# A linear-attention recurrence run seven slots ahead instead of six, with its input loads split and its VectorE and ScalarE order changed

## The reference

```python
for t in range(S):                       # S = 768, D = 40, 4 x 8 heads
    y[:, :, t] = np.einsum('bhd,bhde->bhe', rt, state)
    Sa = np.einsum('bhde,bhe->bhd', state, at)
    state_decay = state * wt[:, :, None, :] - np.einsum('bhd,bhe->bhde', Sa, bt)
    state = state_decay + np.einsum('bhd,bhe->bhde', vt, kt)
```

## Time and profile before

| | |
|---|---|
| median of 3 runs | 1002.68 us (999.1 to 1007.23) |
| the profiled execution | 1005.59 us, its span 1003.9 us |
| busy over the span | PE 82%, DVE 55%, ACT 31%, POOL 25% |
| recurrence | from 0 to about 441 us of the span |
| mean granted TensorE clock | 0.83 of full speed from 104 to 383 us, 0.99 after 435 us |

### The profile page before, as it was taken

One profiled execution on the slowest core, in us unless ns is written; L12 is line 12 of the kernel. 1 busy time (PEld: TensorE's weight loads), 2 busy tenths in 40 slices (PEclk: granted clock), 3 DMA queues, 4 the chain that ended last, 5 costly groups with the idle time before them and its releaser, 6 DMA issues.

```text
span 1003.9 us, 27604 instructions
## 1 busy us (share of the span) xinstructions
PE 826.9 (82%) x11872; PEld 603.9 (60%) x11872; DVE 556.5 (55%) x1235; ACT 312.4 (31%) x739; POOL 252.2 (25%) x524
## 2 busy tenths in 40 slices
PE   2318988897998978859998789997899987899977
PEld 2218888897887978844454555455544545554555
DVE  8686667767776653125436635347355366353464
ACT  3102222223222222212225532235422255312354
POOL 1075856687776876000000000000000000000000
PEclk9999787898777888789999999999999999999999
DMA  3525455565656536232000000100000000000000
GB/s 102 137 57 115 96 131 127 131 147 112 137 121 132 133 73 159 60 101 81 10 31 7 21 14 1 40 1 21 14 7 30 10 12 17 14 1 0 1 21 20
DMA packets 125336, 61.31 MB, mean 61 GB/s; under 512 B 105120, under 2 KB 118048, under 8 KB 123296
## 3 DMA queue, kind: packets, MB, share of 16 engines
q1 hardware_dynamic: 95172, 32.61, 14.5%
q10 hardware_dynamic: 30044, 26.94, 10.4%
HBM read 45.37 MB, written 14.16 MB: 59 GB/s over the span
## 4 chain that ended last, share of the span: by engine, by line
PE 66%; DVE 15%; DMA 7%; ACT 6%; issue 4%; SPq 2%; ACTq 1%; DVEq 0%
PE ps_all L737 9%; PE ps_all L721 8%; PE ps_scan L103 4%; PE ps_all L778 4%; DMA l_by_unit<-l_blocks 3%; PE ps_all L854 3%; PE ps_all L815 3%; PE ps_scan L194 3%; ACT probs L914 3%; PE ps_scan L174 3%; PE ps_all L833 3%; PE ps_all L731 3%; PE ps_all L845 2%; PE ps_all L724 2%; DVE t_update_first L314 2%
## 5 line engine op out<-in xcount | busy, mean ns | idle before, releaser
L314 POOL TENSOR_TENSOR t_update<-l_by_unit,t_by_unit 128x133 f32<-128x133 f32 (+13 forms) x251 | 118.0, 470 | 131.8 <-DVE t_by_unit L316 64.4
L316 POOL TENSOR_TENSOR t_by_unit<-t_by_unit,t_update 128x133 f32<-128x133 f32 (+13 forms) x251 | 128.8, 513 | 19.7
L103 PE MATMUL ps_scan<-decayed_a_and_eye,scaled_then_x 40*128 40x104 f32 x768 | 67.8, 346 | 55.9 <-DVE decayed_a_and_eye L346 55.9
L721 PE MATMUL ps_all<-scaled_then_x,inputs_then_w_up 128*128 128x384 f32 x256 | 91.0, 499 | 15.7 <-DMA scaled_then_x<-y_t 10.0
L103 PEld LDWEIGHTS ps_scan<-decayed_a_and_eye,scaled_then_x 40*128 40x128 f32 x768 | 62.7, 252 | 57.9 <-DVE decayed_a_and_eye L346 42.3
L1005 DVE TENSOR_REDUCE minus_max<-ps_all 128x1 f32<-128x128 f32 (+5 forms) x96 | 54.9, 618 | 75.2 <-PE ps_all L819 75.2
L737 PE MATMUL ps_all<-gated,w_down 128*128 128x384 f32 x256 | 91.1, 499 | 0.0
L721 PEld LDWEIGHTS ps_all<-scaled_then_x,inputs_then_w_up 128*128 128x128 f32 x256 | 48.7, 194 | 52.2 <-issue 12.0
L880 ACT ACTIVATE h<-ps_all 128x384 f32<-128x384 f32 x64 | 28.0, 490 | 148.7 <-PE ps_all L724 148.7
L737 PEld LDWEIGHTS ps_all<-gated,w_down 128*128 128x128 f32 x256 | 46.0, 189 | 44.6 <-issue 19.1
L951 DVE TENSOR_SCALAR conv<-h,w_conv 128x768 f32<-128x768 f32 x32 | 19.9, 621 | 94.7 <-ACT h L880 94.7
(11 more groups left out here) (115 smaller groups left out, 1519.2 us busy)
## 6 DMA issues: line engine op xcount, KB each, us to landing
inputs_then_w_up<-in_x ACTq DMA_DIRECT2D x46, 321.4 KB
r_t_and_v_t<-in_rv ACTq DMA_DIRECT2D x48, 160.0 KB
l_by_unit<-l_blocks SPq DMA_DIRECT2D x24, 256.0 KB, 5.0
uv_and_ruv<-in_v ACTq DMA_DIRECT2D x48, 80.0 KB, 3.0
y_t<-y_out SPq DMA_DIRECT2D x24, 160.0 KB
out<-out_rows SPq DMA_DIRECT2D x24, 160.0 KB, 1.8
l_blocks<-ak_and_l SPq DMA_DIRECT2D x96, 32.0 KB, 2.0
t_blocks<-t_by_unit SPq DMA_DIRECT2D x24, 128.0 KB, 4.7
```

The lines of the kernel that those rows point to most:

```text
L103: last = nc.tensor.matmul(PS[:, o:o + ROWS], weights, AL[c % NK][rows(h), p, :], start=True, stop=True)
L314: return (lambda: eng.tensor_tensor(tmp[:, 0:cols, 0:rest], l[:, s:s + 1, s + 1:BLK].broadcast_to(shape), t[:, 0:cols, s:s + 1].broadcast_ ...
L316: lambda: eng.tensor_tensor(t[:, 0:cols, s + 1:BLK], t[:, 0:cols, s + 1:BLK], tmp[:, 0:cols, 0:rest], ALU.subtract))
L721: nc.tensor.matmul(bank[n][:, 0:HALF], WIN[:, t, cols], XT[:, t, n * HALF:(n + 1) * HALF], start=(t == 0), stop=False)
```

## The change

GA becomes 7, so a chunk is prepared seven slots ahead, the loop has one slot more ahead of slot 0, and one more buffer of three kinds is allocated (by NK and NQK). A chunk's input load becomes three parts with semaphores of their own: w, a, and k with b. On ACT the w part of the next chunk is issued after the copy of x, the a part of this slot's chunk after that of y, the k and b part of the next chunk after `bkn_move`, and the second copy of x (`ZS`) stands ahead of `bkn_move`. On DVE the odd slots have a new order: four solver steps, hm, five solver steps, gm, prefixes, suffixes, bk and the rest. Even slots keep theirs. `solve_first` moves to slot -3, at the same chunks as before.

```diff
-GA = 6
+GA = 7
+FIRST = 4
+PARTS = {"w": slice(0, WCOLS + 1), "a": slice(WCOLS + 1, WCOLS + 1 + HC), "kb": slice(WCOLS + 1 + HC, XCOLS)}
...
-        def load_x(c):
+        def load_x(c, part):
             if c >= 2:
                 act.wait_ge(m["prepped"], c - 1)
             for h in range(2):
-                act.dma_start(INX[c % 2][rows(h), :], in_x[c, h]).then_inc(m[f"inx{c % 2}"], 16)
+                act.dma_start(INX[c % 2][rows(h), PARTS[part]], in_x[c, h][:, PARTS[part]]).then_inc(m[f"{part}{c % 2}"], 16)
...
             if live: move(XS, PX, "x", "x_sb", n)
+            if next_up: load_x(n + GA + 1, "w")
             if live: move(YS, PY, "y", "y_sb", n, -1.0)
-            if 2 <= n + GA + 1 < NT: load_x(n + GA + 1)
+            if soon: load_x(n + GA, "a")
+            if live: move(ZS, PX, "e", "z_sb", n)
             if ahead: bkn_move(c)
-            if live: move(ZS, PX, "e", "z_sb", n)
+            if next_up: load_x(n + GA + 1, "kb")
             if live: u_move(n)
...
-            if prep: prefixes(c)
-            if after: hm(n - 1)
-            if prep: suffixes(c)
-            if n % 2 == 1 and 2 <= (n + GA - 3) // 2 < NPAIR: solve_head((n + GA - 3) // 2)
-            if ahead: gm(g)
-            if n == -2: solve_first()
+            pair = (n + 3) // 2
+            if n % 2 == 1 and 2 <= pair < NPAIR:
+                solve_head(pair, range(0, FIRST))
+                hm(n - 1)
+                solve_head(pair, range(FIRST, HEAD))
+                if ahead: gm(g)
+                if prep: prefixes(c)
+                if prep: suffixes(c)
+            else:
+                if prep: prefixes(c)
+                if after: hm(n - 1)
+                if prep: suffixes(c)
+                if ahead: gm(g)
+            if n == -3: solve_first()
```

More of the change, by code:

```diff
@@ L72, in recurrence @@
              "solved pool_chain set_eye consts set_inx set_dve set_pool arrived go "
-             "inx0 inx1 v0 v1 v2 r0 r1 r2 l_out0 l_out1 l_in t_out t_in0 t_in1 stored0 stored1")
+             "w0 w1 a0 a1 kb0 kb1 v0 v1 v2 r0 r1 r2 l_out0 l_out1 l_in t_out t_in0 t_in1 stored0 stored1")
     m = {n: sem("r_" + n) for n in names.split()}
@@ L266, in scalar @@
         act.wait_ge(m["set_inx"], 2)
-        load_x(1)
+        for part in ("w", "kb", "a"):
+            load_x(1, part)
         act.wait_ge(m["consts"], 4)
@@ L279, in scalar @@
             live, ahead = 0 <= n < NT, 0 <= c < NT
+            soon, next_up = 2 <= n + GA < NT, 2 <= n + GA + 1 < NT
             if live: move(XS, PX, "x", "x_sb", n)
+            if next_up: load_x(n + GA + 1, "w")
             if live: move(YS, PY, "y", "y_sb", n, -1.0)
-            if 2 <= n + GA + 1 < NT: load_x(n + GA + 1)
+            if soon: load_x(n + GA, "a")
+            if live: move(ZS, PX, "e", "z_sb", n)
             if ahead: bkn_move(c)
-            if live: move(ZS, PX, "e", "z_sb", n)
+            if next_up: load_x(n + GA + 1, "kb")
             if live: u_move(n)
@@ L321, in prefixes @@
         def prefixes(c):
-            dve.wait_ge(m[f"inx{c % 2}"], 32 * (c // 2 + 1))
+            dve.wait_ge(m[f"w{c % 2}"], 32 * (c // 2 + 1))
             if c >= 1:
@@ L334, in bk @@
         def bk(c):
+            dve.wait_ge(m[f"kb{c % 2}"], 32 * (c // 2 + 1))
             if c >= 2:
@@ L342, in al @@
         def al(c):
+            dve.wait_ge(m[f"a{c % 2}"], 32 * (c // 2 + 1))
             if c >= NK:
@@ L388, in solve_first, with solve_head @@
                     sub().then_inc(m["solved"], 1)
[L390 to L396, removed]
+        def solve_head(j, steps):
+            if steps.start == 0:
+                dve.wait_ge(m["l_in"], 32 * (j + 1))
+                dve.wait_ge(m["eye"], j + 1)
+                dve.wait_ge(m["solved"], 1)
+                if j >= 3:
+                    dve.wait_ge(m["head"], j - 2)
+            for s in steps:
                 mult, sub = step(nc.vector, LU[j % 2], TS[j % 2], TMD, s)
@@ L527, in sync @@
         sp.wait_ge(m["set_inx"], 1)
-        for h in range(2):
-            sp.dma_start(INX[0][rows(h), :], in_x[0, h]).then_inc(m["inx0"], 16)
+        for part in ("w", "kb", "a"):
+            for h in range(2):
+                sp.dma_start(INX[0][rows(h), PARTS[part]], in_x[0, h][:, PARTS[part]]).then_inc(m[f"{part}0"], 16)
         sp.wait_ge(m["set_pool"], 1)
```

## The result

The changed kernel is **slower, by 1.4%**: median 1020.6 us over 20 runs (1007.95 to 1030.41), the kernel before 1001.7 over 20 (994.47 to 1009.24), ratio 1.014 with a 95% interval of 1.010 to 1.017. Runs more than 1.5% above the fastest of the same kernel, 8 of the 20 here and none of the kernel before, are left out of this and all later ratios; the plain medians give 1.019. Forecast were 980 us and a range that ended at 1001.

The account below looks back on a forecast made before the run. PE work plus low clock was taken as the bound, with DVE's l_in wait lengthening odd slots. Pairs fall from 31.6 to 28.4 us, 29 less; start costs 7.2, slot 18 gives 1: 23 less, 980 us, range 955 to 1001.

Parts of the forecast that it names:

- the first of the odd slots: DVE, odd slots: four solver steps follow al's end at +3.6 directly, take 1.91 us and end at +5.5.
- the 6.0 us that the prediction took off each odd slot: Odd slots: gm starts at g_products' end, +10.6 and not +16.6, so 6.0 us less each at full clock.
- the queue behind the head's wait: Rival: DVE's head still waits for l_in, hm and g_products behind it; about 998 us, 1009 at worst; chance 0.08.
- l_in's waits: DVE's eight waits for l_in, 26.4 us, go; the round trip fits with 2.9 us to spare.
- Late hm: Odd slots: hm runs to +6.8, g_products needing it start at +8.6, so hm is covered, by 1.8 us.
- The clock: TensorE's low clock: of 10.7 low us a pair, 4.0 go and 6.7 stay, costing 3.35; granted clock 0.85 to 0.9.
- a clock that stays up: Rival: nothing is low in odd slots, PE needs 25.0 a pair, POOL's 26.0 binds; 958 us, chance 0.2.
- The second copy of x: On ACT ahead of bkn_move: nothing by itself in even slots, up to 1 us where DVE is late; 0.3 taken.
- ACT's queue with its ten issues: Rival: ACT's DMA issues hold back y and u, 1.9 us a slot, 32.2 a pair; 1014 us, chance 0.1.
- The start: Ahead of slot 0: one slot more stands there and costs 7.2 us.
- The loads of x: At the start: part of chunk 3 behind v and r loads, between 2 less and 2.5 us more, taken as 0.
- The three loads: ACT: six issues for two, same bytes, 0.1 us at worst; taken as nothing.

Follow-up runs that it names:

- e1: Changed kernel with the identity copy (eye_move) moved early in even slots, between the copies of y and x; 988.1 us, 0.986 of the kernel before.
- e8: Changed kernel with the identity copy moved just ahead of the v and r loads, behind the copy of u; 992.3 us, 0.988 of the kernel before.
- e9: Changed kernel with the identity copy a slot later, behind the copy of x and the w part's issues; 1042.3 us, 1.032 of the kernel before.
- e2: Changed kernel with hm ahead of all nine solver steps in odd slots; 996.6 us, 0.992 of the kernel before.
- e11: Changed kernel with the early identity copy, but GA = 6 and solve_first at slot -2; 1029.4 us, 1.022 of the kernel before.
- e7: Changed kernel with the early identity copy and the second copy of x back behind bkn_move; 993.2 us, 0.986 of the kernel before.
- e6: Kernel before with three loads and the second copy of x ahead of bkn_move, at GA = 6 and old DVE order; 1003.9 us, 1.000.
- e5: Changed kernel with the early identity copy, and hm ahead of prefixes in even slots too; 990.1 us, 0.984 of the kernel before.

## Why the prediction was wrong

**The step that failed** is the first of the odd slots: "Four solver steps take 1.91 us (224.56 to 226.47), so to +5.5", counted from al's end at +3.6. It took l_in for the only thing that the head waits for. `solve_head` also waits for `eye_move` (and for earlier solver work of DVE's own, done by then). On ACT it stands at the end of the even slot, behind four issues of v and r. The trace of before had its time, in ACT's order of slot 8:

```profile
218.46 0.63 ACT L245 ACTIVATE t_by_unit<-eye_by_unit 128x512 f32<-128x512 f32 x1 [1.77 <-issue]
```

It ends at 219.09, +6.4 in the prediction's count. Before, the head started at +11.9, so nobody waited. Moved to +3.6 it must wait 2.8 us, and hm, at +5.4, stands behind. With this row the sum is head at +6.4, hm from +8.3 to +9.6, g_products 1.0 us late with a new gap on PE in every odd slot: the mechanism in the trace after. Measured were 3.4 us a head (34.7 us in nine, less the last one's 7.1, in eight). In place of the 6.0 us that the prediction took off each odd slot, 1.2 came off (18.1 to 16.9). The prediction had priced the queue behind the head's wait as a rival, but with l_in as the cause and 0.08 as the chance; the form was right and the waited-for thing was another. e1, e8 and e9, which move nothing but this copy, settle that, and e2 shows that the price is mostly hm behind it.

**What stood.** With that copy in time (e1) the sum comes out: 28.5 us a pair for 28.4, 988 us for 980. Some of that closeness is luck. The clock is low for 8.9 us a pair, where I had 6.7, so that PE is busy 26.9 us for my 26.4; it is idle 1.6 us for my 2.0, and the two errors offset each other. In it:

- l_in's waits went, in the changed kernel and in e1, and e11 has them back at 7.1 us.
- Late hm has a cover of some 2 us (e8 loses nothing that can be measured).
- The clock: 0.85 in e1, at the lower end of the 0.85 to 0.9 that I had named, and odd slots recovered while even ones grew from 13.5 to 15.1 us. The low stretches did move there: 3.0 us low in an odd slot for 7.0 before, 5.9 in an even one for 4.0. The rivals of a clock that stays up, and of POOL as the bound at 26.0, did not come in.
- The second copy of x gives nothing (e7), and ACT's queue with its ten issues did not hold y back enough to matter in e1; that the rival's 1014 us lies near the changed kernel's time is chance.

**What was mis-sized.** The start costs 8.8 to 9.1 us (the changed kernel and e1) for my 7.2: the extra slot is 7.3 of it (77.96 to 85.27), the rest comes later, up to slot 0's mark. The loads of x came late behind v and r at the start as before; I had 0 for it and 0.5 is measured (gm of chunk 3 at 45.76 for 45.18). The three loads, which I took at nothing, are worth 14 to 16 us in the tight order: 28.4 rested on them without my knowing. I had looked only at the bytes, which are equal, and at ACT's idle time; e6 shows the same split worth nothing in the old order. The page DMA: Bandwidth & Descriptors of the Trainium skill (Rules for kernel authors) advises authors to merge many small transfers into a large one, and names 64 KB as the size under which overhead dominates. The parts here, 80 to 160 KB an issue, are above that, so its figure isn't put to the test; its advice, carried on to such sizes, would have cost 1.6% in e1. I also counted 22 waits where the trace has 19; their sum of 13.4 us stands.

**What stays open.** The changed kernel's single runs spread from 1008 us at a mean granted clock of 0.939 to 1030 at 0.917. Low clock and long time go together, but what makes one run fall into more low stretches than another was not tried. No trace shows the 12 us between the changed kernel's profiled execution and its median. Nor was it settled why one load for three costs time, or what keeps e1's even slots at 15.1 us; e5 excludes hm.

## What to carry to other kernels

When an instruction is moved forward, list every semaphore that it waits for and read from the trace when each is set, also those on which nobody has ever waited; the earliest start is the latest of them. Whatever is queued behind the moved instruction pays for the one you forgot. And before a lookahead is counted as won, find what sits at the end of another engine's queue, behind its DMA issues: moving one copy forward by some 2 us (e8) was worth 2.6% here, more than the 1.4% by which e1 beats the kernel before.

## What was not expected of the hardware

The same bytes at the same DMA share (0.60) cost 1.6% more time when they come as one load of 640 KB a slot, two issues of 320 KB, than as three loads in six issues (1.002 for 0.986); in the kernel's old order the split made no difference (e6, 1.000). And a gap of 1.58 us on PE was again followed by 9.5 us at a granted clock of 0.51. From e1 to e9 about half of the time lost per pair (2.7 of 5.5 us) is idle time of PE; the other half is busy time at a lower granted clock (0.76 for 0.85).
